# Three expert tiles without tokens move from the end of the plan to places 1, 3 and 5, and two PSUM banks change roles

## The chip, the cores and the metric

The kernel runs on one core of one Trainium2 chip. The metric is the device time of one execution in microseconds (us). Below, the engines are called PE (TensorE, matrix products), ACT (ScalarE), DVE (VectorE), POOL (GpSimd) and SP (SyncE, which only issues transfers here).

## The reference

Three stages run one after the other: windowed causal attention, a dense block with h - tanh(h), and a mixture of eight experts in which every token goes to one expert. Cut to what matters:

```python
# q, k, v: (4, 8, 576, 64); keys from 63 back to the query itself
attn = softmax(q @ k.T / 8, masked to 0 <= i - j < 64) @ v
x = attn as (2304, 512)
h = x @ w_in                        # 512 -> 2048
x = (h - tanh(h)) @ w_out           # 2048 -> 512
# mixture: 8 experts, one for each token
logits = cosine(x, expert_emb) / tau
expert_idx = argmax(logits); gate = softmax(logits)[expert_idx]
for e in range(8):
    mask = expert_idx == e
    hid = maximum(x[mask] @ w1[e], 0)          # 512 -> 1024
    out[mask] = gate[mask] * (hid @ w2[e])     # 1024 -> 512
```

## The kernel before

Every product is made of three fp32r products (high by high, high by low, low by high; `products`, L1159 to L1164), so each operand is first split into a high part (ACT, a cast) and a low part (DVE, a subtraction).

The first two stages take some 570 us and are one interleaved schedule; they are touched only in POOL's `constants(2)` (L508 to L518), which makes small tables while `w_in` is being split.

The third stage is the one that the change is about. Tokens are routed to slots of a table in DRAM, sorted by expert. Each expert's tokens are cut into tiles of 128, the last one padded. The number of tiles in the program is fixed at NTILE = (2304 + 8 * 127) // 128 = 25, enough for the worst routing. How many of them hold tokens depends on the inputs. A plan made by DVE (L986 to L1015) says for each place s of the 25: which expert (`plan[0]`), whether the expert changes at s (`plan[1]`), which of two weight slots is used (`plan[2]`), and whether the tile is live, that is, has tokens (`plan[3]`). Before, all live tiles come first. `rows` (L1000), used by an indirect load on POOL (L566), says where in the table the tokens of each place stand. A place without tokens reads rows that hold the index T, a padding row.

The loop over places (`experts`, L295) is unrolled for s = 0 to 3 and from 20 on, and a hardware loop of four places a round between. In step s each engine does, in this order:

- PE: the first product of s (24 matmuls, or for a tile that is not live only waits and two semaphore increments, L1323 to L1328); transposes of the gathered tokens of s+1 (L1294); the second product of s-1 (24 matmuls, or a wait and an increment); eight transposes of `hid` of s (L1340).
- ACT: `hTh` of s-1, rounding of `w2` of s and of `w1` of s+1 when the expert changes there (L689, four pieces), `relu` of s (L734), `xgh` of s+1 (L754), the scaled result `y` of s-1 (L764).
- DVE: `hTl` of s-1 (L1055), the low parts of `w2` of s and `w1` of s+1 (L966), `take_ids` of s+2 (L1031, L1032), `xgl` of s+1 (L1063).
- POOL: the scatter of `y` of s-2 to the output (L587), the gather of the tokens of s+2 (L577), which waits for `take_ids` of s+2.
- SP: `fetch(s)`: 4 transfers of `w1` and 4 of `w2`, carried out only where the expert changes at s. Each waits until the same piece of place s-1 has been split (or been passed over).

Each engine works its list strictly in order. Only the two matrix products are left out for a tile that is not live: gather, transposes, `relu`, splits, `y` and scatter are done for all 25.

The experts of the 22 live tiles here change at live tiles 2, 4, 7, 11, 15, 17 and 19 (counted from 0): these are the places at which ACT rounds new weights. The places 22, 23 and 24 have no tokens.

Of the kernel before, what the change touches and what calls it, by code (L numbers as in the profile page):

```python
# [9 lines left out]
ALU = mybir.AluOpType  # L10
AX = mybir.AxisListType.X
ds = bass.ds

P = 128
# [20 lines left out]
def build(nc, q, k, v, w_in, w_out, emb, tau, w1, w2, out):  # L35
    B, H, S, D = q.shape
    T, DM, F = B * S, H * D, w_in.shape[1]
    E, _, F2 = w1.shape
    KC, FC, F2C = DM // P, F // P, F2 // P

# [15 lines left out]
    NTILE = (T + E * (P - 1)) // P  # L56
    REGION = T
    ROWS = E * REGION + P
# [6 lines left out]
    with ExitStack() as ctx:  # L65
        def sb(name, shape, dt=F32, scope=ctx):
            return scope.enter_context(nc.sbuf_tensor(name, shape, dt))

        def sem(name):
            return ctx.enter_context(nc.semaphore(name))  # L70

        def sems(name, n):
            return [sem(f"{name}{i}") for i in range(n)]

        banks = ctx.enter_context(nc.psum_tensor("banks", [P, 8, BANK], F32))
# [21 lines left out]
        plan = sb("plan", [P, 4, NTILE], I32)  # L97
        tiles18 = sb("tiles18", [P, E, MAXT])
        tri8 = sb("tri8", [P, E, E])
        jcol = sb("jcol", [P, NTILE])  # L100
        pcol = sb("pcol", [P, 1])
        notfirst = sb("notfirst", [P, E])
        changes = sb("changes", [P, NTILE + 1])
        en1 = sb("en1", [E, 3])
        enroot = sb("enroot", [E, 1])

# [60 lines left out]
        phase2 = ctx.enter_context(ExitStack())  # L167
# [23 lines left out]
        ended = sb("ended", [P, NTILE, E], scope=phase2)  # L191
        moved = sb("moved", [P, NTILE, E], scope=phase2)
        c8 = [sb(f"c8_{i}", [P, E], scope=phase2) for i in range(8)]
        experts_ended = sb("experts_ended", [P, NTILE], scope=phase2)
        row = [sb(f"row{i}", [P, 1], scope=phase2) for i in range(2)]
        rows = sb("rows", [P, 1], I32, phase2)

        mstep, dstep = sem("mstep"), sem("dstep")
        ident_made, masks_made, pads_zeroed, consts_made = sem("ident_made"), sem("masks_made"), sem("pads_zeroed"), sem("consts_made")
# [23 lines left out]
        rows_planned, tabs_loaded, tabs_transposed, ids_ready, ids_taken = (sem(n) for n in (  # L223
            "rows_planned", "tabs_loaded", "tabs_transposed", "ids_ready", "ids_taken"))
# [35 lines left out]
        psJ = banks[:, 0, :]  # L260
        psG = [banks[:, i, :] for i in (0, 1)]
        psHT = [banks[:, i, :] for i in (2, 3)]
        psY = [banks[:, i, :] for i in (4, 6)]
        psXG = banks[:, 5, :]

        q_blocks = q.rearrange("b h (i p) d -> p (b h i) d", p=WINDOW)
        k_blocks = k.rearrange("b h (i p) d -> p (b h i) d", p=WINDOW)
# [45 lines left out]
        def chained(eng, semaphore, base=0):  # L313

            done = [0]

            def then(instruction):
                done[0] += 1
                instruction.then_inc(semaphore, 1)
                eng.wait_ge(semaphore, base + done[0])  # L320
            return then
# [124 lines left out]
        def _(pool):  # L446

            alone = chained(pool, mstep)
            alone(pool.memset(ident[:], 0.0))
            alone(pool.affine_select(out=ident[:], in_=ident[:], compare_op=ALU.not_equal, fill=1.0, base=0,  # L450
                                     pattern=[[-1, P]], channel_multiplier=1))
# [3 lines left out]
            for h in range(2):  # L455
                m = mask[h * WINDOW:(h + 1) * WINDOW]
                alone(pool.affine_select(out=m, in_=m, compare_op=ALU.is_ge, fill=MASKED, base=-1,
                                         pattern=[[1, P]], channel_multiplier=-1))
                alone(pool.affine_select(out=m, in_=m, compare_op=ALU.is_ge, fill=MASKED, base=WINDOW,
                                         pattern=[[-1, P]], channel_multiplier=1))  # L460
# [32 lines left out]
            def constants(part):  # L493
                if part == 0:
                    alone(pool.memset(power[:], 0.5))
                    alone(pool.memset(plain_ones[:], 1.0))
                    alone(pool.affine_select(out=plain_tri[:], in_=plain_ones[:], compare_op=ALU.is_gt, fill=0.0, base=0,
                                             pattern=[[1, P]], channel_multiplier=-1))
                    alone(pool.memset(added[:], 0.0))
                    for exact, plain in ((ones, plain_ones), (tri, plain_tri), (running, added)):  # L500
                        alone(pool.tensor_copy(exact[:], plain[:]))
                if part == 1:
                    for st in range(ST):

                        alone(pool.iota(pair[st][:, 0:1], [[0, 1]], base=P * st - TB, channel_multiplier=1, allow_small_or_imprecise_dtypes=True))
                    alone(pool.iota(em8[:], [[0, ST], [1, E]], base=-E, channel_multiplier=0, allow_small_or_imprecise_dtypes=True))
                    alone(pool.iota(rowbase[:], [[0, ST], [REGION, E]], base=0, channel_multiplier=0, allow_small_or_imprecise_dtypes=True))
                if part == 2:  # L508
                    alone(pool.iota(tiles18[:], [[0, E], [P, MAXT]], base=0, channel_multiplier=0, allow_small_or_imprecise_dtypes=True))
                    alone(pool.memset(tri8[:], 1.0))  # L510
                    alone(pool.affine_select(out=tri8[:], in_=tri8[:], compare_op=ALU.is_ge, fill=0.0, base=0,
                                             pattern=[[1, E], [-1, E]], channel_multiplier=0))
                    alone(pool.iota(jcol[:], [[1, NTILE]], base=0, channel_multiplier=0, allow_small_or_imprecise_dtypes=True))
                    alone(pool.iota(pcol[:], [[0, 1]], base=0, channel_multiplier=1, allow_small_or_imprecise_dtypes=True))
                    alone(pool.memset(notfirst[:], 1.0))
                    alone(pool.memset(notfirst[:, 0:1], 0.0))
                    alone(pool.memset(changes[:, 0:1], 0.0))
                    pool.sem_inc(consts_made, 1)  # L518

            def scatter_slots(m):  # L520
                pool.wait_ge(slotted, m + 1)
                pool.wait_ge(table_cleared, 32)
                for st in range(ST):
                    pool.indirect_dma_start(out=table, out_offset=bass.IndirectOffsetOnAxis(ap=slot[:, st:st + 1], axis=0),
                                            in_=pair[st][:], in_offset=None).then_inc(scattered, 16)

            constants(0)
            for j in range(FIRST + 5):
                if 3 <= j < FIRST + 3:
# [12 lines left out]
            for n in range(NBLK):  # L542
                for c, s in steps(n):
                    if n == 0 and c + 2 < FC:
                        split_w_in(c + 2)
                    pieces(s)
                    pieces(s + 1)
                    if n == 0 and c in (3, 5):
                        constants(1 if c == 3 else 2)
                    if n == 0 and c == 6:  # L550
                        pool.wait_ge(en_squared, 1)
                        pool.tensor_tensor(enroot[:], en1[:, 0:1], power[0:E, 0:1], ALU.pow).then_inc(en_rooted, 1)
                    if n > 0 and c == 9:
                        pool.wait_ge(squared, ST * n)
                        pool.tensor_tensor(norm[:], ss[:], power[:], ALU.pow).then_inc(rooted, 1)
                    if n > 0 and c == 12:
                        scatter_slots(n - 1)
# [223 lines left out]
        def _(dve):  # L781
# [203 lines left out]

            dve.wait_ge(totals_ready, 1)  # L986
            then = chained(dve, planstep)
            count, tiles, ends, moves, starts, filled, passed, jumped = (t[:] for t in c8)
            then(dve.tensor_copy(count, psN))
            then(dve.tensor_tensor(cmp18[:], count.unsqueeze(2).broadcast_to((P, E, MAXT)), tiles18[:], ALU.is_gt))  # L990
# [1 line left out]
            then(dve.tensor_tensor(prod8[:], tiles.unsqueeze(1).broadcast_to((P, E, E)), tri8[:], ALU.mult))  # L992
            then(dve.tensor_reduce(ends, prod8[:], AX, ALU.add))
            then(dve.tensor_scalar(moves, tiles, -float(P), float(REGION), ALU.mult, ALU.add))
            then(dve.tensor_scalar(passed, ends, pcol[:, 0:1], None, ALU.is_le))
            then(dve.tensor_tensor(jumped, passed, moves, ALU.mult))
            then(dve.tensor_reduce(row[0][:], jumped, AX, ALU.add))
            then(dve.tensor_scalar(row[1][:], row[0][:], 1.0 / P, pcol[:, 0:1], ALU.mult, ALU.add))

            dve.tensor_scalar(rows[:], row[1][:], float(E * REGION // P), None, ALU.min).then_inc(rows_planned, 1)  # L1000


            then(dve.tensor_tensor(ended[:], jcol[:].unsqueeze(2).broadcast_to((P, NTILE, E)), ends.unsqueeze(1).broadcast_to((P, NTILE, E)), ALU.is_ge))
            then(dve.tensor_reduce(experts_ended[:], ended[:], AX, ALU.add))
            then(dve.tensor_scalar(plan[:, 0, :], experts_ended[:], float(E - 1), None, ALU.min))
            then(dve.tensor_tensor(starts, ends, tiles, ALU.subtract))
            then(dve.scalar_tensor_tensor(out=filled, in0=tiles, scalar=0.0, in1=notfirst[:], op0=ALU.is_gt, op1=ALU.mult))
            then(dve.tensor_tensor(ended[:], jcol[:].unsqueeze(2).broadcast_to((P, NTILE, E)), starts.unsqueeze(1).broadcast_to((P, NTILE, E)), ALU.is_ge))
            then(dve.tensor_tensor(moved[:], ended[:], filled.unsqueeze(1).broadcast_to((P, NTILE, E)), ALU.mult))
            then(dve.tensor_reduce(changes[:, 1:NTILE + 1], moved[:], AX, ALU.add))  # L1010
            then(dve.tensor_tensor(plan[:, 1, :], changes[:, 1:NTILE + 1], changes[:, 0:NTILE], ALU.subtract))
            then(dve.tensor_copy(plan[:, 2, :], changes[:, 1:NTILE + 1]))
            then(dve.tensor_scalar(plan[:, 2, :], plan[:, 2, :], 1, None, ALU.bitwise_and))
            then(dve.tensor_scalar(plan[:, 3, :], jcol[:], ends[:, E - 1:E], None, ALU.is_lt))
            dve.sem_inc(planned, 1)  # L1015
            low_first_w1([0])

# [383 lines left out]
```

## Time and profile before

| | us |
|---|---|
| median of 3 runs | 893.06 |
| lowest, highest | 890.51, 893.79 |
| the profiled execution, its own time | 894.78 |
| span in its trace | 893.0 |
| PE busy in the span | 831.4 (93%) |
| ACT busy, DVE busy | 362.3 (41%), 398.3 (45%) |
| mean granted clock, as a share of 2.4 GHz | 0.964 |

All times inside the trace are counted from the start of the span. The time lies 1.8 us above the span. A row of the timeline gives the start, the duration, the engine and line, the operation, the tile that it writes and those that it reads, the number of instructions merged, and in brackets the idle time before it with what ended it. SPq and POOLq are issues of transfers.

### The profile page before, as it was taken

The page shows a single profiled execution, that of the slowest core. Times are in us where ns is not written, and L with a number is a line of the kernel's source. Part 1 is how long each engine was busy: PE and PEld are TensorE (multiplying, and loading weights), DVE is VectorE, ACT ScalarE, POOL GpSimd, SP SyncE. Part 2 cuts the span into 40 slices and gives each one's busy share as a digit, 9 for nine tenths or more (in the row PEclk, how much of TensorE's full clock was granted, in tenths as well). Part 3 has the DMA queues.
Part 4 walks back from the last instruction along what each step waited for, and adds up shares of the span by engine and source line. Part 5 has one row for each costly group of instructions (what it writes and reads, how often), then busy time and mean ns, then how long its engine had stood idle before and what let it go on. Part 6 is the DMA issues. An engine that isn't in the chain of part 4 may idle for free. (4 is left out here: it accounts for less than half of the span.)

```text
span 893.0 us, 16016 instructions
## 1 busy us (share of the span) xinstructions
PE 831.4 (93%) x4496; PEld 727.1 (81%) x4497; DVE 398.3 (45%) x1205; ACT 362.3 (41%) x880; POOL 201.7 (23%) x288
## 2 busy tenths in 40 slices
PE   3679999999999999999999999668999999999992
PEld 3679998889999989988889999557888888888871
DVE  3436655445444544444443333555435251455412
ACT  2525554333433343334333222515535262555423
POOL 2636651112111211121112001120111111111111
PEclk9879999999999999999999999869999999999996
DMA  5494112211211112112003400116634251655210
GB/s 126 106 277 128 39 45 63 69 26 32 56 55 24 34 41 78 40 27 79 23 1 56 168 2 0 36 37 213 228 124 142 85 182 41 235 212 214 60 38 23
DMA packets 101299, 77.34 MB, mean 87 GB/s; under 512 B 79132, under 2 KB 80289, under 8 KB 101234
## 3 DMA queue, kind: packets, MB, share of 16 engines
q1 hardware_dynamic: 96610, 65.20, 24.7%
q0 software_dynamic: 4624, 11.32, 4.1%
q8 instruction: 34, 0.56, 0.3%
q14 instruction: 31, 0.25, 0.1%
HBM read 142.39 MB, written 11.44 MB: 172 GB/s over the span
## 5 line engine op out<-in xcount | busy, mean ns | idle before, releaser
L1162 PE MATMUL banks<-xh,win_h 128*128 128x384 f32 x384 | 137.4, 358 | 1.8 <-POOL xl L482 1.8
L1164 PE MATMUL banks<-xh,win_l 128*128 128x384 f32 x384 | 130.8, 341 | 0.0
L1163 PE MATMUL banks<-xl,win_h 128*128 128x384 f32 x384 | 130.4, 340 | 0.0
L870 DVE TENSOR_TENSOR gf<-banks,gf 128x384 f32<-128x384 f32 x96 | 53.5, 557 | 157.3 <-ACT gf L652 157.3
L652 ACT ACTIVATE gf<-banks 128x384 f32<-128x384 f32 x96 | 47.2, 491 | 184.2 <-PE banks L1164 184.2
L1162 PE MATMUL banks<-wout_h,gh 128*128 128x512 f32 x288 | 119.1, 414 | 0.0
L1164 PE MATMUL banks<-wout_h,gl 128*128 128x512 f32 x288 | 113.7, 395 | 0.0
L1163 PE MATMUL banks<-wout_l,gh 128*128 128x512 f32 x288 | 112.7, 391 | 0.0
L472 POOL TENSOR_TENSOR sm<-sm,rr 128x384 f32<-128x384 f32 x48 | 41.9, 874 | 305.7 <-DVE rr L821 305.7
L874 DVE TENSOR_TENSOR gl<-gf,gh 128x384 fp32r<-128x384 f32 x96 | 55.1, 574 | 112.7 <-ACT gh L659 108.1
L659 ACT CAST gh<-gf 128x384 fp32r<-128x384 f32 x96 | 49.2, 512 | 128.9 <-PE banks L1164 127.7
L1162 PEld LDWEIGHTS banks<-xh,win_h 128*128 128x128 f32 x384 | 73.3, 191 | 2.7 <-POOL xl L482 2.1
L1163 PEld LDWEIGHTS banks<-xl,win_h 128*128 128x128 f32 x384 | 73.4, 191 | 0.6
L1055 DVE TENSOR_TENSOR hTl<-banks,hTh 128x512 fp32r<-128x512 f32 x50 | 32.3, 686 | 92.2 <-ACT hTh L745 92.1
L1164 PEld LDWEIGHTS banks<-xh,win_l 128*128 128x128 f32 x384 | 73.2, 191 | 0.0
L1162 PE MATMUL banks<-w1h,xgh 128*128 x176 | 71.2, 404 | 2.1 <-DVE xgl L1063 1.0
L1162 PE MATMUL banks<-w2h,hTh 128*128 x176 | 70.8, 402 | 0.9 <-DVE hTl L1055 0.9
L1164 PE MATMUL banks<-w1h,xgl 128*128 x176 | 69.2, 393 | 0.0
L1164 PE MATMUL banks<-w2h,hTl 128*128 x176 | 68.9, 391 | 0.0
L1163 PE MATMUL banks<-w1l,xgh 128*128 x176 | 68.7, 390 | 0.0
L1163 PE MATMUL banks<-w2l,hTh 128*128 x176 | 68.6, 390 | 0.0
L607 ACT ACTIVATE sm<-sm,nmx 128x128 f32<-128x128 f32 x144 | 55.8, 391 | 21.0 <-DVE nmx L810 20.9
(185 smaller groups left out, 1487.4 us busy)
## 6 DMA issues: line engine op xcount, KB each, us to landing
w1raw<-in_moe_w_dram SPq DMA_DIRECT2D x104, 512.0 KB
w2raw<-in_moe_w_dram SPq DMA_DIRECT2D x104, 512.0 KB
vw<-in_v_dram SPq DMA_DIRECT2D x48, 96.0 KB, 2.7
x_rows<-x SPq DMA_DIRECT2D x6, 768.0 KB, 3.8
wout_raw<-in_moe_w_out_dram SPq DMA_DIRECT2D x4, 1024.0 KB, 6.8
win_raw<-in_moe_w_in_dram SPq DMA_DIRECT2D x3, 1024.0 KB, 8.2
qk<-in_q_dram SPq DMA_DIRECT2D x30, 96.0 KB, 2.7
qk<-in_k_dram SPq DMA_DIRECT2D x30, 96.0 KB, 2.7
```

The source lines that it names most:

```text
L472: pool.tensor_tensor(sm[g % 4][:], sm[g % 4][:], rr[:, g % 4, :].unsqueeze(2).broadcast_to((P, GB, P)), ALU.mult).then_inc(normed, 1)
L607: last = act.activation(sm[g % 4][:, u, :], sm[g % 4][:, u, :], ACT.Exp, bias=nmx[:, g % 4, u:u + 1], scale=-1.0, accum_out=rs[:, g % 4, u ...
L652: act.activation(gf[c % 2][:], psH[c % 2], ACT.Tanh).then_inc(tanh_ready, 1)
L659: act.copy(gh[c % 2][:], gf[c % 2][:]).then_inc(g_high, 1)
L870: dve.tensor_tensor(gf[c % 2][:], psH[c % 2], gf[c % 2][:], ALU.subtract).then_inc(g_ready, 1)
L874: dve.tensor_tensor(gl[c % 2][:], gf[c % 2][:], gh[c % 2][:], ALU.subtract).then_inc(g_split, 1)
L1055: dve.tensor_tensor(hTl[:, part, :], psHT[half].rearrange("p (k t) -> p k t", k=KC), hTh[:, part, :], ALU.subtract).then_inc(hT_split, 1)
L1162: pe.matmul(to, sh, mh, start=start, stop=False)
L1163: pe.matmul(to, sh, ml, start=False, stop=False)
L1164: return pe.matmul(to, sl, mh, start=False, stop=stop)
```

## The change

The plan counts the tiles without tokens (`idle_tiles` = 25 less the live ones). Place j is idle if j is odd and fewer than `idle_tiles` odd places lie before it; `place_of[j]` is j less the idle places up to j, and takes the place of j in all comparisons with the experts' ends and starts. With 3 idle tiles these are the places 1, 3 and 5. They keep the expert of the live tile before them. A row of an idle place is pushed beyond the table's last region by adding ROWS before the minimum, so that it still reads padding. The order of the live tiles stays. The live tiles 0, 1, 2, 3, 4, 5, ... stand at the places 0, 2, 4, 6, 7, 8, ..., so that the expert changes at the places 4, 7, 10, 14, 18, 20 and 22.

POOL makes two more tables. The chain of DVE between the token counts and `rows` gets six more instructions, and the rest of the plan up to `planned` three more. The PSUM bank of the odd tiles' second product becomes 5 in place of 6, and the one of the transposed tokens 6 in place of 5. Nothing in the loop over the places is edited.

```diff
-        psY = [banks[:, i, :] for i in (4, 6)]
-        psXG = banks[:, 5, :]
+        psY = [banks[:, i, :] for i in (4, 5)]
+        psXG = banks[:, 6, :]
...
+                    alone(pool.iota(halves[:], [[1, (NTILE + 1) // 2], [0, 2]], base=0, channel_multiplier=0, allow_small_or_imprecise_dtypes=True))
+                    alone(pool.memset(odd_rows[:], 1.0))
+                    for i in range(2):
+                        alone(pool.affine_select(out=odd_rows[:, i, :], in_=odd_rows[:, i, :], compare_op=ALU.is_ge, fill=0.0, base=i - 2,
+                                                 pattern=[[-2, (NTILE + 1) // 2]], channel_multiplier=1))
...
+            then(dve.tensor_reduce(idle_before_row[:], odd_rows[:], AX, ALU.add))
...
-            then(dve.tensor_scalar(passed, ends, pcol[:, 0:1], None, ALU.is_le))
+            then(dve.tensor_scalar(idle_tiles[:], ends[:, E - 1:E], -1.0, float(NTILE), ALU.mult, ALU.add))
+            then(dve.tensor_scalar(row_idle[:], idle_before_row[:], idle_tiles[:, 0:1], None, ALU.min))
+            then(dve.tensor_tensor(place_of_row[:], pcol[:], row_idle[:, 1:2], ALU.subtract))
+            then(dve.tensor_tensor(row_is_idle[:], row_idle[:, 1:2], row_idle[:, 0:1], ALU.subtract))
+            then(dve.tensor_scalar(passed, ends, place_of_row[:, 0:1], None, ALU.is_le))
...
-            then(dve.tensor_scalar(row[1][:], row[0][:], 1.0 / P, pcol[:, 0:1], ALU.mult, ALU.add))
-            dve.tensor_scalar(rows[:], row[1][:], float(E * REGION // P), None, ALU.min).then_inc(rows_planned, 1)
-            then(dve.tensor_tensor(ended[:], jcol[:].unsqueeze(2).broadcast_to((P, NTILE, E)), ends.unsqueeze(1).broadcast_to((P, NTILE, E)), ALU.is_ge))
+            then(dve.tensor_scalar(row[1][:], row[0][:], 1.0 / P, place_of_row[:, 0:1], ALU.mult, ALU.add))
+            then(dve.scalar_tensor_tensor(out=row[2][:], in0=row_is_idle[:], scalar=float(ROWS), in1=row[1][:], op0=ALU.mult, op1=ALU.add))
+            dve.tensor_scalar(rows[:], row[2][:], float(E * REGION // P), None, ALU.min).then_inc(rows_planned, 1)
+            then(dve.tensor_scalar(idle[:], halves[:], idle_tiles[:, 0:1], None, ALU.min))
+            then(dve.tensor_tensor(place_of[:], jcol[:], idle[:, 1:NTILE + 1], ALU.subtract))
+            then(dve.tensor_tensor(is_idle[:], idle[:, 1:NTILE + 1], idle[:, 0:NTILE], ALU.subtract))
+            then(dve.tensor_tensor(ended[:], place_of[:].unsqueeze(2).broadcast_to((P, NTILE, E)), ends.unsqueeze(1).broadcast_to((P, NTILE, E)), ALU.is_ge))
...
-            then(dve.tensor_scalar(plan[:, 3, :], jcol[:], ends[:, E - 1:E], None, ALU.is_lt))
+            then(dve.tensor_scalar(plan[:, 3, :], is_idle[:], -1.0, 1.0, ALU.mult, ALU.add))
```

## Rows read from the trace of the kernel before

**Rows 1.** The page's costliest groups: one of the expert products

```profile
L1162 PE MATMUL banks<-w1h,xgh 128*128 x176 | 71.2, 404 | 2.1 <-DVE xgl L1063 1.0
```

**Rows 2.** PE's timeline from the third stage's start: start us, duration

```profile
592.54 2.06 PE L1277 MATMUL banks<-w1h,ones 128*128 128x512 f32 x4
...
601.17 1.07 PE L1340 MATMUL banks<-ident,hid 128*128 128x128 f32 x8
...
615.86 1.14 PE L1340 MATMUL banks<-ident,hid 128*128 128x128 f32 x8 [0.91 <-ACT hid L734]
...
618.01 0.49 PE L1162 MATMUL banks<-w1h,xgh 128*128 x1 [1.01 <-issue]
...
629.52 1.03 PE L1340 MATMUL banks<-ident,hid 128*128 128x128 f32 x8
...
641.81 1.03 PE L1340 MATMUL banks<-ident,hid 128*128 128x128 f32 x8
642.60 0.47 PE L1162 MATMUL banks<-w1h,xgh 128*128 x1
```

**Rows 3.** The timeline of all engines around the last live tile

```profile
868.83 0.97 POOL L577 DMA_INDIRECT xg<-x_rows,ids  x1 [3.01 <-DVE ids L1032]
...
871.21 0.69 ACT L764 ACTIVATE y<-banks,gate 128x512 f32<-128x512 f32 x1 [2.20 <-PE banks L1164]
...
872.98 0.66 PE L1294 MATMUL banks<-ident,xg 128*128 128x128 f32 x4 [0.93 <-DMA xg<-x_rows,ids]
873.05 1.02 POOL L587 DMA_INDIRECT out_dram<-y,ids  x1 [3.25 <-issue]
```

**Rows 4.** The chain that ended last: start us, us, what

```profile
882.43 0.70 DVE hTl L1055
...
884.73 0.98 POOL out_dram L587
```

**Rows 5.** The answer on the output tensor: how long its scatters take

```profile
DMA to landing us min/median/max: 2.1/2.8/5.5
```

**Rows 6.** The other engines' timeline in the third stage's first steps

```profile
599.81 0.95 POOL L577 DMA_INDIRECT xg<-x_rows,ids  x1 [8.24 <-DVE ids L1032]
...
617.23 1.09 ACT L745 CAST hTh<-banks 128x512 fp32r<-128x512 f32 x2
...
618.35 3.90 ACT L689 CAST w2h<-w2raw 128x1024 f32 x4
...
619.85 4.63 DVE L966 TENSOR_TENSOR w2l<-w2raw,w2h 128x1024 f32 x4 [0.69 <-ACT w2h L689]
...
624.40 0.15 DVE L1031 COPY gate<-gates_all 128x1 f32<-128x1 f32 x1
...
626.54 2.47 SPq L414 DMA_DIRECT2D w1raw<-in_moe_w_dram  x4
...
633.21 3.90 ACT L689 CAST w1h<-w1raw 128x1024 f32 x4 [1.85 <-issue]
```

**Rows 7.** DVE's and POOL's timeline while the plan is made

```profile
578.05 0.15 DVE L1000 TENSOR_SCALAR rows<-row 128x1 int32<-128x1 f32 x1
...
581.36 0.24 DVE L1014 TENSOR_SCALAR plan<-jcol,c 128x25 int32<-128x25 f32 x1
...
583.62 0.97 POOL L566 DMA_INDIRECT tabs<-slots,rows  x1 [4.71 <-issue]
```

**Rows 8.** POOL and PE in the dense stage's first block

```profile
87.18 1.30 POOL L491 TENSOR_TENSOR win_l<-win_raw,win_h 128x512 fp32r<-128x512 f32 x1
...
94.50 0.42 PE L1162 MATMUL banks<-xh,win_h 128*128 128x384 f32 x1
```

**Rows 9.** Windows: stretch, busy times by engine, granted clock, DMA share, GB/s

```profile
596.00:596.25 0.25, 0.25 (x3) 0.21 (x2) 0.25 (x1) 0.00 (x0) 0.00 (x0) 0.92 0.00 0
...
617.00:618.00 1.00, 0.00 (x1) 0.00 (x0) 0.63 (x2) 1.00 (x3) 0.92 (x1) 1.00 0.17 64
...
875.75:876.00 0.25, 0.25 (x4) 0.18 (x3) 0.00 (x0) 0.25 (x2) 0.00 (x0) 0.86 0.00 0
```

More of the change, by code:

```diff
@@ L103, in build @@
         changes = sb("changes", [P, NTILE + 1])
+        halves = sb("halves", [P, NTILE + 1])
+        odd_rows = sb("odd_rows", [P, 2, (NTILE + 1) // 2])
         en1 = sb("en1", [E, 3])
@@ L194, in build @@
         experts_ended = sb("experts_ended", [P, NTILE], scope=phase2)
-        row = [sb(f"row{i}", [P, 1], scope=phase2) for i in range(2)]
+        row = [sb(f"row{i}", [P, 1], scope=phase2) for i in range(3)]
         rows = sb("rows", [P, 1], I32, phase2)
+        idle_before_row = sb("idle_before_row", [P, 2], scope=phase2)
+        idle = sb("idle", [P, NTILE + 1], scope=phase2)
+        is_idle = sb("is_idle", [P, NTILE], scope=phase2)
+        row_is_idle = sb("row_is_idle", [P, 1], scope=phase2)
+        idle_tiles = sb("idle_tiles", [P, 1], scope=phase2)
+        place_of_row = sb("place_of_row", [P, 1], scope=phase2)
+        place_of = sb("place_of", [P, NTILE], scope=phase2)
+        row_idle = sb("row_idle", [P, 2], scope=phase2)
         mstep, dstep = sem("mstep"), sem("dstep")
@@ L1007, in _ @@
             then(dve.scalar_tensor_tensor(out=filled, in0=tiles, scalar=0.0, in1=notfirst[:], op0=ALU.is_gt, op1=ALU.mult))
-            then(dve.tensor_tensor(ended[:], jcol[:].unsqueeze(2).broadcast_to((P, NTILE, E)), starts.unsqueeze(1).broadcast_to((P, NTILE, E)), ALU.is_ge))
+            then(dve.tensor_tensor(ended[:], place_of[:].unsqueeze(2).broadcast_to((P, NTILE, E)), starts.unsqueeze(1).broadcast_to((P, NTILE, E)), ALU.is_ge))
             then(dve.tensor_tensor(moved[:], ended[:], filled.unsqueeze(1).broadcast_to((P, NTILE, E)), ALU.mult))
```

## The prediction

> **What bounds the kernel now.** I read the page first: PE is busy 93% of the span, and each of the eight matmul groups of the expert stage has 176 members [rows 1]. A live tile has 8 of each group (4 pieces of the contraction by 2 halves), so 22 tiles are live and 25 - 22 = 3 places are idle: the change does act on these inputs. Then PE's timeline: once the stage runs, the transposes of `hid` of one live tile begin 12.29 us after those of the one before (629.52, 641.81), with no idle time between. So PE sets the pace there, and it is 0.79 us from these eight transposes to the next product (641.81 to 642.60); the four of `xg` are half of that, 0.4, and each of the two products is (12.29 - 0.8 - 0.4) / 2 = 5.6 us [rows 2]. Last, the timeline around the end and the chain that ended last. The last live tile's `y` is scaled at 871.21 and its scatter goes out at 873.05; then three idle places still follow one another through transposes, `relu`, split, `y` and scatter, and the last scatter goes out at 884.73 [rows 3, 4]. That is 11.7 us in which no expert product runs. At the front PE loses a little too: before the third live tile it waits 0.91 and 1.01 us for work behind the first newly loaded weights [rows 2].
>
> **What it takes away.** The tail of idle places: 884.73 - 873.05 = 11.7 us [rows 3, 4]. The live tail stays as it was, since the last live tile's second product had an idle place behind it before as well. An idle scatter writes nothing and a live one does, and landings range from 2.1 to 5.5 with a median of 2.8 [rows 5]; I take 0.2 us of loss there, from 0 to 0.7 (2.8 - 2.1).
>
> **What it adds in front.** An idle place leaves out two products, which are what hides the other engines' work, and leaves in everything else. I follow the clock of the trace of before, with these pieces: a gather takes 872.98 - 868.83 = 4.1 us from issue until PE transposes [rows 3]; a half of `relu` or `hTh` 0.6, `xgh` 0.6 (1.09 for two halves [rows 6], the others taken alike), `y` 0.7 [rows 3], a split on DVE 0.7 [rows 4]; four pieces of weights are rounded in 3.9 us, and their low parts are done 619.85 + 4.63 - 618.35 = 6.15 us after the rounding began, with `take_ids` right behind (624.40) [rows 6].
>
> Step 1 is idle. The gather of place 2 goes out at 599.81, so PE, done with `hid` of tile 0 at 602.24 [rows 2, 6], waits until 603.9, and the second product of place 0 starts at 604.5 (0.4 of transposes, 0.2 to start). Step 2 is live, expert unchanged: 5.6 + 0.8, first product from 610.9 to 616.5. Step 3 is idle: ACT must do half of `relu` (617.2), `xgh` (617.8), `y` (618.5) and half of `hTh` (619.1), DVE a half of `hTl` (619.8), and the second product of place 2 starts at 620.2 and ends at 625.8.
>
> Meanwhile the first new weights, now for place 4, are late. SP may fetch `w1` of place 4 only when DVE has passed over place 3, in its step 2, at about 614, and issues near 616.2. From the issue at 626.54 to the rounding's start at 633.21 was 6.7 us, and its last piece did not wait [rows 6], so by 623 to 624 the pieces are there. ACT comes to them at 619.6 + 1.85 (the pause before the same rounding, 633.21 [rows 6]) = 621.5, ends at 625.4 and only then does `relu` (626.5); DVE ends at 621.5 + 6.15 = 627.6, then `take_ids` and `xgl`, 628.5. So first product of place 4 at about 629.0, to 634.6. It stands behind three queues here (ACT's rounding, DVE's low parts, then `xgl`), as it did before, but with 5.6 us less of products over it.
>
> Step 4 rounds `w2` of place 4: ACT after `xgh`, `y` and `hTh` of place 3 at 629.5; DVE's low parts end at 635.6. Behind them in DVE's queue is `take_ids` of place 6, behind that POOL's gather (636.0), which lands at 640.1. Place 5 is idle and covers nothing: the second product of place 4 starts at 640.7 instead of near 636, and ends at 646.3. Place 6, live, has its first product from 647.1 to 652.7, and place 7 changes expert once more: ACT begins at 648.2 + 2.1 = 650.3, DVE ends at 656.5, `xgl` 657.4, first product of place 7 at 657.9.
>
> Place 7 is live tile 4. Before, its first product started at 642.60 [rows 2]. The state behind it is the same, so the front costs 657.9 - 642.6 = 15.3 us. Of this, 3 x (0.8 + 0.4) = 3.6 are transposes of idle places, the rest are waits. The lower bound takes 3.4 us for a gather (its 0.97 of issue, then 2.4; the first gathers of the stage are no more exact) and with it 13.5; the upper one takes 1 us more for each of two places at which gather and weights share the DMA engines, 17.3. After place 7 no idle place follows, and the pace is 12.3 again.
>
> **What it adds elsewhere.** The six instructions before `rows` and three more before `planned` are short like those around them: (581.36 - 578.05) / 12 = 0.28 us each, and 0.15 to 0.24 where they are as small as L1000 and L1014, so 1.3 and 1.9 us. `rows` comes at 578.2, but the load that uses it goes out at 583.62, held by the slot scatters [rows 7], so 4 us hide it. `planned` moves from 581.6 to 583.5; of those who wait for it, SP's first fetches are held by DVE's low parts anyway, and PE is in its warming matmuls. I take 0; with the cover gone it is 1.9. POOL's four extra instructions take about 1 us: they stand before the split that ends at 88.5, and PE starts on those columns at 94.50 [rows 8], so 6 us hide them, and 1 us is the price otherwise. The banks change roles only between stages whose reads are long over: 0.
>
> **The clock.** After the last dense product ended at 871.0, the granted clock stayed full through sparse transposes until 875.75 to 876.00, where it fell (0.86 is the mix) to 1.2 GHz, 4.9 us later; it did not fall in the 3.1 us between the products around 615.86 and 618.01 (1.00). It came back at about 596.0, after matmuls running from 592.54 and some before [rows 2, 9]; half speed over 3.5 to 4.2 us costs 1.7 to 2.1 us. After the change the distances between dense products are 3.8 (step 1), 3.7 (step 3), 3.2, 6.1 (step 5) and 5.2 (step 7). The 6.1 is longer than the one that lost the clock, the 5.2 is on the edge, the others are nearer the one that kept it. So I count one loss, 2.0 us, with bounds of none and two (4.1).
>
> The Trainium skill ("TensorE: Matmul & The Clock Gate", "HAM oscillation — how this bites in real kernels") says that waits between bursts of matmuls send the array back to half clock, and that this is paid again at each wait. The trace agrees that a sparse stretch does it (875.75 [rows 9]); that waits as short as 3.7 us do, no row here shows. By that page the waits in steps 1 and 3 would be paid as well.
>
> **The sum.** -11.7 + 0.2 + 15.3 + 2.0 = +5.8 us. The profiled execution took 894.78, 1.7 above the median of 893.06; on the median the sum gives 898.9.
>
> **The rivals.**
> Clock kept: the same without the 2.0, +3.8, 896.9. For it speaks that transposes run inside each gap; against it, they ran in the tail too.
> Clock lost at the four long gaps: +3.8 + 4 x 2.0 = +11.8, 904.9. Against it: the gap at 615.86 kept its clock with almost as much sparse time. This is what the cited page would make of it.
> Faster, because the idle steps are hidden: they give SP time, and the weights that PE waited for before (0.91 + 1.01) come under other work. If PE lost only the 3.6 us of transposes and won the 1.9, the sum were -11.7 + 0.2 + 3.6 - 1.9 = -9.8, 883.3. It needs the gathers to be back before PE asks, and ACT's rounding not to stand before `relu`; the order of the lists speaks against it. It decides the sign from a front cost below 11.5 us, and makes 0.5% from one below 7.
> The plan is exposed: `planned` or `rows` late by 1.9 with everything else as above, +7.7, 900.8. The 4 us before the load at 583.62 speak against it.
> That nothing changes (no idle tile) is excluded by [rows 1].
>
> **How the numbers follow.** One loss of clock 0.33 (898.9), clock kept 0.22 (896.9), two to four losses 0.17 (900.9 to 904.9), plan exposed 0.05, a front cost of 7 to 11.5, as between the hidden case and mine, 0.11 (888.6 to 893.1), hidden 0.12 (about 883 to 888). What a measurement of this kernel can tell from no change is 0.5%, 4.5 us: below 888.6 or above 897.5. Faster is the hidden case, 0.12. Slower takes the losses of clock and the exposed plan, 0.55, less a tenth of them for a front at its lower bound, plus a tenth from the clock-kept case at its upper: 0.52. The rest, 0.36, is the same. The range leaves out most of the hidden case below and the four losses above: 889 to 904. The likeliest's own range is 897 to 901 by the bounds of the front.
>
> **What would show it.** In the trace after: the last scatter within 2 us of the last live `y`, and no sparse stretch of three steps before it; the first product of the fifth live tile near 658; PE idle before `xg` at steps 1 and 5, ended by the gather; ACT's first `w1` rounding at about 621 to 622 without a wait for DMA, and PE's transposes of `hid` waiting for `relu` behind it; `tabs` still loaded at about 583.6; the clock below 1.00 in the stretch 640 to 645. The prediction is wrong if gathers come back well before 4 us, if the unchanged steps' pauses on ACT and DVE are longer than I took (then each idle step costs more), or if the clock is lost at every gap.

## The result and the profile after

The changed kernel takes 908.03 us (median of 4, 905.57 to 911.48) against 893.15 for the kernel before: ratio 1.0173, 95% interval 1.015 to 1.0195. The forecast was 898.9, with a range of 889 to 904. The direction was right, the size was not: 14.9 us instead of 5.8.

PE's timeline of the changed kernel over the first steps of the expert stage, cut to the rows that matter, which answers to [rows 2]. The transposes of `xg` (gathered tokens) are L1319 here, those of `hid` L1365; a row of L1187 is the first of the 24 matmuls of a product.

```profile
600.71 0.60 PE L1319 MATMUL banks<-ident,xg 128*128 128x128 f32 x4
601.15 1.07 PE L1365 MATMUL banks<-ident,hid 128*128 128x128 f32 x8
604.00 0.66 PE L1319 MATMUL banks<-ident,xg 128*128 128x128 f32 x4 [1.77 <-DMA xg<-x_rows,ids]
605.61 0.69 PE L1187 MATMUL banks<-w2h,hTh 128*128 x1 [0.96 <-issue]
612.80 1.03 PE L1365 MATMUL banks<-ident,hid 128*128 128x128 f32 x8
619.13 0.60 PE L1319 MATMUL banks<-ident,xg 128*128 128x128 f32 x4
619.57 1.07 PE L1365 MATMUL banks<-ident,hid 128*128 128x128 f32 x8
622.91 1.11 PE L1319 MATMUL banks<-ident,xg 128*128 128x128 f32 x4 [2.27 <-DMA xg<-x_rows,ids]
624.55 0.79 PE L1187 MATMUL banks<-w2h,hTh 128*128 x1 [0.52 <-issue]
632.48 1.03 PE L1365 MATMUL banks<-ident,hid 128*128 128x128 f32 x8
638.84 0.60 PE L1319 MATMUL banks<-ident,xg 128*128 128x128 f32 x4
639.57 1.09 PE L1365 MATMUL banks<-ident,hid 128*128 128x128 f32 x8
645.97 1.11 PE L1319 MATMUL banks<-ident,xg 128*128 128x128 f32 x4 [5.32 <-DMA xg<-x_rows,ids]
647.84 0.79 PE L1187 MATMUL banks<-w2h,hTh 128*128 x1 [0.76 <-issue]
656.08 1.03 PE L1365 MATMUL banks<-ident,hid 128*128 128x128 f32 x8
662.44 0.60 PE L1319 MATMUL banks<-ident,xg 128*128 128x128 f32 x4
664.60 1.09 PE L1365 MATMUL banks<-ident,hid 128*128 128x128 f32 x8 [1.56 <-ACT hid L750]
667.25 0.79 PE L1187 MATMUL banks<-w1h,xgh 128*128 x1 [1.56 <-DVE xgl L1088]
```

The idle steps 1, 3 and 5 begin behind the transposes of `hid` at 601.15, 619.57 and 639.57. With its first product left out, PE waits there for gathered tokens: 1.77, 2.27 and 5.32 us. Then comes one second product, and these last too long: 605.61 to 612.80 is 7.2 us, 624.55 to 632.48 is 7.9, 647.84 to 656.08 is 8.2, where 5.6 is the length at full clock. The windows say why. Their columns are the stretch, its length, the busy times of PE, its weight loads, DVE, ACT and POOL, the granted clock, the DMA share and GB/s. The first four stretches are those three products and the beginning of place 7's first one, the last is a piece of the first:

```profile
605.60:612.80 7.20, 7.19 (x25) 5.75 (x25) 0.91 (x3) 0.91 (x2) 0.94 (x1) 0.76 0.14 36
624.50:632.50 8.00, 7.95 (x25) 6.34 (x26) 5.62 (x7) 4.61 (x6) 0.96 (x1) 0.68 0.97 365
647.80:656.10 8.30, 8.27 (x25) 6.51 (x26) 0.62 (x1) 0.00 (x0) 0.44 (x1) 0.65 0.77 284
667.20:673.00 5.80, 5.75 (x18) 4.65 (x19) 5.32 (x6) 4.36 (x5) 1.91 (x2) 0.71 0.19 62
608.50:609.00 0.50, 0.50 (x2) 0.39 (x2) 0.00 (x0) 0.00 (x0) 0.00 (x0) 0.50 0.74 197
```

The granted clock, third number from the right, is 0.76, 0.68, 0.65 and 0.71 on average: each of the four runs for some time at 1.2 GHz (0.50 in the last row) and gets 2.4 back on the way.

What DVE and POOL do ahead of the longest wait:

```profile
636.26 4.63 DVE L982 TENSOR_TENSOR w2l<-w2raw,w2h 128x1024 f32 x4 [1.09 <-ACT w2h L705]
641.35 0.15 DVE L1056 COPY gate<-gates_all 128x1 f32 x1 [0.46 <-DVEq L1070]
...
642.49 0.97 POOL L593 DMA_INDIRECT xg<-x_rows,ids  x1 [7.22 <-DVE ids L1057]
```

The row numbers for place 6 are taken (`take_ids`) from 641.35 on, behind the low parts of `w2`; the gather leaves at 642.49 and PE can use it at 645.97, 3.5 us later.

The plan's chain, against [rows 7]:

```profile
579.33 0.15 DVE L1022 TENSOR_SCALAR rows<-row 128x1 int32<-128x1 f32 x1
...
583.37 0.18 DVE L1039 TENSOR_SCALAR plan<-is_idle 128x25 int32<-128x25 f32 x1
...
584.18 1.60 POOL L582 DMA_INDIRECT tabs<-slots,rows  x1 [5.22 <-issue]
```

`rows` and the plan come 1.3 and 2.0 us later, and the load that uses `rows` starts 0.6 later. The end, against [rows 3, 4]:

```profile
896.90 0.69 ACT L780 ACTIVATE y<-banks,gate 128x512 f32<-128x512 f32 x1 [6.26 <-PE banks L1189]
898.38 0.98 POOL L603 DMA_INDIRECT out_dram<-y,ids  x1 [6.92 <-ACT y L780]
```

The last live `y` comes 896.90 - 871.21 = 25.7 us later than before, and nothing follows its scatter. The last scatter of all moved from 884.73 to 898.38, 13.65 us, and the span's rest behind it grew from 8.3 to 8.8 us: together the 14.2 us between the spans (907.2, 893.0).

### The profile page after: what moved, and what is told of

The parts are those of the page before. It is cut to its first block and busy times, and to the rows that moved or that the text cites. A ratio compares the mean times of both kernels' runs of the same rounds, so it can differ in the third digit from the quotient of the medians.

```text
span 907.2 us, 16024 instructions
## 1 busy us (share of the span) xinstructions
PE 835.9 (92%) x4496; PEld 729.1 (80%) x4497; DVE 400.0 (44%) x1214; ACT 362.5 (40%) x880; POOL 203.5 (22%) x292
## 5 line engine op out<-in xcount | busy, mean ns | idle before, releaser
L1187 PE MATMUL banks<-xh,win_h 128*128 128x384 f32 x384 | 137.3, 357 | 1.8 <-POOL xl L492 1.8
L1187 PE MATMUL banks<-wout_h,gh 128*128 128x512 f32 x288 | 119.1, 414 | 0.0
L1187 PE MATMUL banks<-w2h,hTh 128*128 x176 | 73.7, 418 | 3.5 <-issue 2.2
L1187 PEld LDWEIGHTS banks<-xh,win_h 128*128 128x128 f32 x384 | 73.3, 191 | 2.7 <-POOL xl L492 2.1
L1187 PE MATMUL banks<-w1h,xgh 128*128 x176 | 71.5, 406 | 2.1 <-DVE xgl L1088 2.1
L1188 PE MATMUL banks<-w2l,hTh 128*128 x176 | 71.2, 405 | 0.0
L1189 PE MATMUL banks<-w2h,hTl 128*128 x176 | 71.2, 404 | 0.0
```

The costliest lines, as they stand in the source:

```text
L1187: pe.matmul(to, sh, mh, start=start, stop=False)
L1188: pe.matmul(to, sh, ml, start=False, stop=False)
L1189: return pe.matmul(to, sl, mh, start=False, stop=stop)
```

## The experiments

Each ratio is against the kernel before, run beside it on the same chip; 0.001 is 0.9 us. In brackets stands its 95% interval. The edits are shown shortened, some in words.

**1. The parts that move no place.** All additions stay, but the idle places are pushed to the end:

```diff
-pool.iota(halves[:], ..., base=0, ...)
+pool.iota(halves[:], ..., base=-20, ...); then max(halves, 0)
-base=i - 2          # odd_rows
+base=i - 42
-plan[3] = 1 - is_idle
+plan[3] = jcol < ends[E - 1]
```

> The changed kernel with all its added instructions, tables and bank roles, but with the three idle places left at the end of the plan (22, 23, 24). Theory of the front (idle places cost PE's waits and its clock in steps 1 to 7): this runs as the kernel before, 893, within 1 us. Rival of the plan and the banks (the added instructions, the later load of the token table or the banks cost several us): 896 to 900. The trace after shows the load of the token table only 0.6 us later, so I expect 893 to 894.

0.9994 (0.9981 to 1.0007). Tables, nine instructions and the banks' roles together cost nothing that can be measured. The whole difference comes from where the idle places stand.

**2. What the idle tail is worth.** The kernel before with `NTILE = 22`.

> The kernel before with 22 places in all instead of 25, so that there is no idle place at all (it leaves out nothing for these inputs, but would not hold every routing). It measures what the idle tail is worth: my sum says 11.7 us less a slower last landing of 0.2 to 0.7: 881.5 to 882. A rival, by which the tail of idle places lies partly under the landing of the last live scatter, gives 884 to 886.

0.9855 (0.9817 to 0.9892), 12.9 us (9.6 to 16.3). The term of 11.7 was sound; these few runs can't tell the two apart.

**3. The clock.** Dummy matmuls behind the left-out first product:

```diff
                     pe.sem_inc(hid_ready, 1)
+                    for _ in range(10):
+                        pe.matmul(banks[:, 7, :], ones[:], ones[:].unsqueeze(1).broadcast_to((P, 4, P)), start=True, stop=True)
```

> The changed kernel with ten dummy matmuls of 512 columns (about 2.2 us at full clock) in PE's list at each idle place, before it waits for the next gathered tokens. Theory of the clock (the four products after the gaps ran 1.6, 2.3, 2.6 and 1.6 us too long because the clock had fallen, 8 us in all): if most of the losses are avoided, 908 falls by 4 to 7 us to 901 to 904, with the products back at 5.6 us. Rival (the products are slow for another reason, as memory or bank traffic): they stay slow and the time is 908 or, by the dummies that outlast a wait, 909.

1.012 (1.006 to 1.0181): the sign is as the clock's theory says, but the interval is wide and touches that of the changed kernel (1.015 to 1.0195). The traces are clearer. The windows of this kernel, over the same four products as above:

```profile
602.80:608.30 5.50, 5.50 (x26) 4.51 (x25) 0.69 (x1) 0.58 (x1) 0.94 (x1) 1.00 0.18 48
620.00:625.60 5.60, 5.60 (x28) 4.59 (x27) 5.05 (x7) 4.58 (x6) 0.00 (x0) 1.00 1.02 364
641.10:646.70 5.60, 5.58 (x25) 4.58 (x26) 0.06 (x1) 0.00 (x0) 0.65 (x1) 1.00 0.79 267
657.80:663.50 5.70, 5.66 (x19) 4.58 (x20) 5.21 (x6) 4.35 (x5) 1.90 (x2) 0.74 0.17 51
```

Three products are back at 5.6 us and a clock of 1.00, with the same bank, the same weights and the DMA engines as busy (a share of 1.02 in the second against 0.97): what had slowed them was the clock, and not memory or bank traffic. The fourth, which has no dummies ahead, still pays. From tile 0's first product to the fifth live tile's it is 657.84 - 591.60 = 66.2 us here and 667.25 - 595.12 = 72.1 in the changed kernel, 5.9 less.

With 14 dummies there and 6 behind the left-out second product:

> The changed kernel with fourteen dummy matmuls behind each left-out first product and six behind each left-out second one; nothing else moved. With ten behind the first alone the ratio was 1.012 and one product pair (place 7) still ran at half clock. Theory of the clock: all products of the steps 0 to 7 at full clock, 1.6 us less and the rest as there: 1.010. If the dummies themselves get in the way of the transposes: 1.013 or more.

1.010 (1.0074 to 1.0126), clear of the changed kernel by some 6.5 us. The number is the one that the theory gave, but its reason did not come true: place 7's first product was to run at full clock, and it did not.

```profile
661.80:667.50 5.70, 5.70 (x18) 4.56 (x19) 5.20 (x6) 4.32 (x5) 1.86 (x2) 0.70 0.21 54
```

So the hit is partly luck. Between the two marks it is 661.80 - 593.57 = 68.2 us, 2.0 more than with ten dummies: they take room themselves.

**4. The gathers, two tries that failed.** `take_ids` of s+2 at the head of DVE's step:

```diff
             def expert_step(r, i):
+                take_ids(r, i, 2)
                 low_hT(r, i)
...
-                take_ids(r, i, 2)
```

> The changed kernel with DVE's choice of the row numbers of place s+2 moved to the head of its list in a step, ahead of the low parts of the weights. Theory of the queue (the gather for place 6 is late because its row numbers stand behind 4.6 us of low parts): the wait of 5.3 us before the tokens of place 6 goes, the one of 2.3 us before place 4 shrinks, and the time falls by 5 to 8 us (one lost clock with it), to 900 to 903. Rival (PE would wait there anyway for the hidden tile's split or the weights): less than 2 us.

1.0396 (1.0367 to 1.0426). The same behind `low_hT`:

> The changed kernel with DVE's choice of row numbers for place s+2 between the low part of hid and the low parts of the weights (the first try put it ahead of both, where it waits for a scatter that has not landed and holds everything behind it). Theory of the queue: PE's wait for the tokens of place 6 (5.3 us) falls under 1 us, the product behind it keeps its clock, and the time falls by 6 to 9 us against the changed kernel, to a ratio of 1.007 to 1.011. Rival (the choice is held by the scatter here too): the ratio stays above 1.015 and DVE waits for a landing in each step.

1.0401 (1.038 to 1.0423); and with dummies on top:

> The same order of DVE's list and, at each idle place, ten dummy matmuls behind the left-out first product and six behind the left-out second one. Theory of the clock and the queue together: no product of the first eight steps runs at 1.2 GHz; what stays are the idle places' transposes (3.6 us) and the waits for relu, rounding and splits. I expect a ratio of 1.000 to 1.005 with the kernel before. Rival (most of the front's price is neither clock nor gather): 1.008 or more.

1.0396 (1.0375 to 1.0416). All three are 20 us worse than the changed kernel. The waits of the second try (who for whom: us in total, times, longest):

```profile
DVE gate L1056 <- DMA out_dram<-y,ids: 51.5, 21, 5.9
...
PE banks L1187 <- DVE xgl L1088: 19.1, 7, 6.0
```

`take_ids` reuses a buffer that a scatter still reads. At its old place that scatter has mostly landed (the changed kernel's DVE waits for it at 646.14, for 2.74 us); moved up, DVE waits for it in 21 steps, and everything behind it in the list, low parts and `xgl`, is late for PE. The rival stated for the second try was right; the expectation for the first had not thought of it. These runs say nothing on the gather for place 6.

**5. The gathers, without touching DVE.** Eight places unrolled, and the first ten gathers read the whole table of row numbers:

```diff
-            for i in range(4):
-                step(0, i)
+            for i in range(8):
+                step(i // 4, i % 4)
...
-                hold(pool, ids_taken, s + 1)
+                pool.wait_ge(ids_ready, 1)              # where s < 10
...
-in_offset=bass.IndirectOffsetOnAxis(ap=ids[buf][:, 0:1], axis=0)
+in_offset=bass.IndirectOffsetOnAxis(ap=ids_all[:, s:s + 1], axis=0)
```

> The changed kernel with eight places unrolled before the loop instead of four, and the gathers of the first ten places reading their row numbers straight from the table, so that they don't stand behind DVE's list at all. The tries before moved DVE's choice and made it wait for scatters in every step; this moves no one else. Theory of the gather: PE's waits for tokens (1.8, 2.3 and 5.3 us before places 2, 4 and 6) go; PE then waits for the split of hid instead, 2.0, 2.1 and 4.7 us earlier than now: 8.8 us less, ratio 1.0173 - 0.0099 = 1.007, and lower if fewer clocks are lost. Rival (the gathers are not what PE waits for last): 1.015 or more.

1.0063 (1.0041 to 1.0085), where the control, the same edit on the kernel before, is near 1:

> The kernel before with the unrolled eight places and the direct gathers of the first ten, nothing moved: the control for the run direct_ids. If these edits only take away waits for gathers, and none binds in the kernel before: ratio 0.999 to 1.001. If the unrolling changes the pace by itself, it is off by more than 0.002 and the gathers' share has to be corrected by that.

0.9991 (0.9979 to 1.0004). So earlier tokens take 1.0173 - 1.0063 = 0.011, some 10 us, from the change's cost. PE's timeline at steps 1, 5 and 7 of the run with places moved, then the windows of the products behind:

```profile
598.58 1.07 PE L1370 MATMUL banks<-ident,hid 128*128 128x128 f32 x8
601.15 0.63 PE L1324 MATMUL banks<-ident,xg 128*128 128x128 f32 x4 [1.50 <-DVE xgl L1093]
602.80 0.50 PE L1192 MATMUL banks<-w2h,hTh 128*128 x1 [1.02 <-DVEq L1075]
...
637.43 0.49 PE L1192 MATMUL banks<-w2h,hTh 128*128 x1 [1.02 <-DVEq L1075]
...
650.97 0.60 PE L1324 MATMUL banks<-ident,xg 128*128 128x128 f32 x4
...
655.35 0.79 PE L1192 MATMUL banks<-w1h,xgh 128*128 x1 [1.45 <-DVE xgl L1093]
```

```profile
602.80:608.40 5.60, 5.60 (x24) 4.61 (x25) 0.91 (x3) 1.14 (x3) 0.00 (x0) 1.00 0.00 1
637.40:644.60 7.20, 7.17 (x24) 5.74 (x25) 0.81 (x3) 1.35 (x3) 0.30 (x1) 0.76 0.51 167
655.30:661.00 5.70, 5.65 (x18) 4.56 (x19) 5.36 (x6) 4.64 (x5) 1.78 (x2) 0.71 0.39 135
```

No wait for tokens is left, but each idle step still has one of 1.4 to 1.6 us for `xgl` or PE's own sequencer, and 1.02 before the product. All four gaps between dense products are shorter (4.7, 4.5, 4.7 and 4.4 us), and two of the four clock losses are gone. But they are not gone by length alone: the shortest, 650.97 to 655.35, still lost it. With dummies on top:

> The same with ten dummy matmuls behind each left-out first product and six behind each left-out second one. Theory of clock and gather together: 1.007 less some 0.006 to 0.008 for the clock: 0.999 to 1.002. Rival (clock and gather don't add up, since the dummies fill waits that are gone): 1.005 or more, with PE's transposes of hid starting later than in the run without dummies.

1.0059 (1.0035 to 1.0084): this missed. In its trace the four products run at full clock, but the stretch between the two marks is 653.70 - 590.06 = 63.6 us, against 655.35 - 592.59 = 62.8 without dummies: what the clock gives back the dummies take, as the rival said. (Counted on to the next transposes of `hid`, behind the last slow product, the two runs are 75.1 and 75.8 us.)

**6. The price of a place.** Lists of places written into the two tables in place of 1, 3, 5 (in words):

```diff
-halves[k] = k // 2
+halves[k] = number of idle places below k, from the list     # memsets
```

First places 9, 14 and 23, each between live neighbours:

> The changed kernel with the idle places at 9, 14 and 23 in place of 1, 3 and 5: apart from each other and not next to a change of expert. Theory: an idle place there costs 1.2 us of transposes and 1.0 to 1.5 us of waiting for the split of hid, its neighbours are live and cover gather and relu, and the clock stays full; 3 x 2.5 = 7.5 us against the 11.7 of the tail: ratio 0.995 (about 887). Rival (an idle place costs 5 us or more wherever it stands, since the products that it leaves out hide the other engines' work): 1.004 or more.

1.0014 (1.0002 to 1.0026): neither theory's number. PE's timeline around place 9:

```profile
700.02 1.03 PE L1370 MATMUL banks<-ident,hid 128*128 128x128 f32 x8
...
722.87 0.60 PE L1324 MATMUL banks<-ident,xg 128*128 128x128 f32 x4
```

Without an idle place the `xg` transposes of the step after next begin, at the pace of [rows 2], 12.29 + 6.36 = 18.65 us after the `hid` transposes (6.36 is a block of `hid` transposes and a first product, 0.79 and 5.57). It takes 22.85, so an idle place costs 4.2 us here, with the clock at 1.00 throughout; I had said 2.5. At the end it costs 3.9. Moving it gains nothing even where it harms least.

One idle place at 14, two at the end, so that live tile 15's new weights come two places behind it:

> Only one idle place moved, to 14, the other two at the end. Theory: minus one third of the tail (3.9 us) plus 2.5 us: ratio 0.998. Rival of the same price everywhere (5 us or more): 1.001 or more. The trace is to show how long PE goes without a dense product around place 14: 3 us or less and a granted clock of 1.00.

1.0051 (1.0033 to 1.007), where my theory said 0.998: the rival holds. It is worse than three spaced ones.

```profile
760.24 1.03 PE L1370 MATMUL banks<-ident,hid 128*128 128x128 f32 x8
...
778.20 1.96 PE L1370 MATMUL banks<-ident,hid 128*128 128x128 f32 x8 [3.02 <-ACT hid L755]
788.00 0.60 PE L1324 MATMUL banks<-ident,xg 128*128 128x128 f32 x4
```

The same distance is 27.76 us, a price of 9.1: `relu` stands behind the rounding of the new `w1` (3.02), which the left-out products no longer cover, and the clock goes (the transposes take 1.96). Nor was the stretch without a dense product 3 us or less, as expected, but 6.5 (774.58 to 781.05). Place 1 alone:

> Only one idle place moved, to 1; the other two at the end. Theory (the front's price adds up place by place): the changed kernel lost 2 to 3 us of waiting, 1.2 of transposes and 1.6 of clock at place 1, less the 1.0 that the kernel before waits there too, against 3.9 of tail: +0 to +2 us, ratio 1.000 to 1.002. Rival (the first new weights come one place later in this order, so that the idle place hides the wait for them): 0.997 or less. Other rival (any idle place ahead of the new weights makes their whole chain late): 1.005 or more.

1.0031 (1.0018 to 1.0044), between the theory (up to 1.002) and the last rival (1.005 or more), so some 6.7 us for the place, in place of the 3.9 in the tail. Its trace shows the clock lost after place 1 and again behind the new weights, where PE waits for `relu` and `xgl`:

```profile
615.99 0.60 PE L1324 MATMUL banks<-ident,xg 128*128 128x128 f32 x4
617.78 1.14 PE L1370 MATMUL banks<-ident,hid 128*128 128x128 f32 x8 [1.19 <-ACT hid L755]
620.33 0.79 PE L1192 MATMUL banks<-w1h,xgh 128*128 x1 [1.41 <-DVE xgl L1093]
```

Three such places at the front cost 25.7 us, 8.6 each.

**7. The tail itself.** The kernel before, with `relu`, the split of `hid` and its transposes passed over at an idle place (`If` on `plan[3]`, increments in the `Else`):

> The kernel before (idle places at the end), in which ACT, DVE and PE pass over relu, the split of hid and its transposes at an idle place, with semaphore increments in their stead; gather, split of the tokens, scaling and scatter stay. The tail is 11.7 us now and the run without any idle place was 12.9 us faster. Theory (the tail is the chain relu, transposes, split of each idle place): it shrinks to about 6 us, ratio 0.994. Rival (the added branches cost the live places as much, or the chain of branches alone takes 3.9 us a place): 1.000 or more.

1.0008 (0.9993 to 1.0023). The scatter of the last live tile and that of the last idle one:

```profile
870.48 1.02 POOL L587 DMA_INDIRECT out_dram<-y,ids  x1 [2.52 <-issue]
...
882.00 0.98 POOL L587 DMA_INDIRECT out_dram<-y,ids  x1 [1.96 <-ACT y L776]
```

11.5 us, as before (11.7). Leaving out that work alone, at the price of a test and a branch on each engine, shortens the tail by nothing that counts. Whether the branches cost as much as the work or the work was never in the way, this run can't tell. Then every engine leaves the whole step:

```diff
             for s in range(4 * rounds, NTILE + 1):
-                step(s // 4, s % 4)
+                with eng.If(eng.value_load(plan[0:1, 3, ds(s - 1, 1)], min_val=0, max_val=1)):
+                    step(s // 4, s % 4)
```

and likewise SP's `fetch(s)` under the test of s, POOL's scatter under that of s-2 and its gather under that of s-1, with the final waits inside.

> The kernel before, in which every engine passes over a whole step from step 20 on when the tile of the step before it is idle, so that the three idle places at the end cost one test of a register each; SP waits for its transfers before the next fetch there. It still holds every routing. Theory (the tail is the chain from engine to engine, mostly branches and register loads, not the work in it): the time comes close to the run without any idle place (ratio 0.9855), 0.985 to 0.989. Rival (the tests themselves, about 1 us each on every engine, make a chain as well): 0.995 or more.

0.989 (0.987 to 0.991), 881.94 us. By the ratios it beats the kernel before by 10 us and the changed one by 25. The last scatter of its trace, in the chain that ended last:

```profile
869.94 1.01 POOL out_dram L600
```

It is the last live tile's, with no idle one behind it. The span ends at 880.7, 10.8 us later, where it was 8.3 in the kernel before and in the run with 22 places: that is most of the 3 us by which this run stays above the latter. Only this routing was run; that the edit holds the others follows from its tests and wasn't measured.

## Why the prediction was wrong, by its own steps

**What bounds, and the tail taken away** (-11.7 + 0.2): right. Without idle places the kernel gains 12.9; the changed kernel has none of that tail.

**The front at full clock** (15.3): right in kind and nearly in size. The last live `y` is 25.7 us late; the four slow stretches are 1.6 + 2.4 + 2.7 + 1.6 us too long (the last from 667.25 to the next transposes of `hid`), two blocks of `xg` transposes 0.5 each, 9.3 in all; that leaves 16.4. Most waits stand where the prediction put them: tokens of places 2 and 6, `relu` behind the rounding and `xgl` behind the low parts at place 7. The wait for the tokens of place 4 is one that it did not have. The gather for place 6 was to leave at 636.0 and left at 642.5, since the steps ahead had run late, and took 3.5 us instead of 4.1. The slow products hide part of this: the wait of 2.4 us before the first product of place 4 (629.0 in the forecast, less 625.8 and 0.8) didn't appear; the product ahead of it ended only at 632.48 and lasted 2.4 longer. ACT's first rounding for place 4 began at 623.29 in place of 621.5 and waited three times for its transfers, 1.2 us in all; this too the slow product hid. The lower bound of 13.5 doesn't come out of its own pieces: 0.7 less for each of the two gathers on the path gives 13.9.

**The clock** (2.0): this step failed. I put the gaps between dense products at 3.8, 3.7, 3.2, 6.1 and 5.2 us and counted one loss of the clock, 2.0 us. The gaps were 4.9, 5.4, none, 9.0 and 4.8, all four lost the clock, and together this cost 9.3 us. Two errors led there. First, the two short gaps came out too short, by 1.1 and 1.7 us. I gave PE 0.2 us to start the product behind the tokens where it idles 0.5 to 1.0 (605.61, 624.55, 647.84). And the gather for place 4 is missing from the working: DVE comes to its row numbers only at 618.06, 2.6 us after the low part of `hid`, and PE waits for the tokens until 622.91. Second, I drew the line at the one gap that I had seen lose its clock, with nothing measured between 3.1 and 4.9. The rival "clock lost at the four long gaps" (904.9; two to four losses had 0.17 of the chance) is what happened. It is 3.1 us short of the median: 1.3 for its 2.0 a loss, which was 2.3 on average, 1.1 for the front, and the rest is the difference between the profiled execution and the median. In the same way the forecast of +5.8 becomes the +14.2 between the two spans: 7.3 by the clock, 1.1 by the front. Dummies in the gaps took 4.7 us off by the ratios and 5.9 by the traces, of the 7.7 that the three losses in their reach had cost.

The rule of the Trainium skill that stood beside it ("TensorE: Matmul & The Clock Gate", "HAM oscillation — how this bites in real kernels"), that each wait between bursts is paid anew, is borne out by these four products, though not by every run: of the four gaps between dense products in the run `direct_ids`, 4.4 to 4.7 us long, two kept the clock. Weighed higher than one gap of the trace before, the rule would have moved the likeliest case to 905.

**Plan, tables, banks** (0): right, 0.9994. **The clock kept, the hidden case, the exposed plan:** none of them occurred. The faster rival fails on what it named itself: the gathers were not back and the rounding stood before `relu`.

**What stays open.** Why each execution of the changed kernel differs more than one of before (905.57 to 911.48; the slowest had the lowest mean clock, 0.954) wasn't tried beyond that. The start of the stage moves from trace to trace as well: tile 0's first product starts between 590.1 and 595.1, which is why stretches between two marks are compared above. In what parts the 3.9 us of an idle place in the tail divide between branches, register loads, gathers and the work itself is not shown. Shown is only that passing over `relu`, transposes and split by branches gains nothing, and that passing over whole steps does.

## What to carry to other kernels

A placeholder in a pipeline costs what its neighbours no longer hide: here 4.2 us between live tiles, 9.1 ahead of a change of weights, 8.6 each for the three at the front, 3.9 at the end, although its own work on PE is 1.2. Before an empty unit of work is moved, ask what the work that it leaves out was covering, and count the clock for every stretch that it makes sparse, including those just above the longest that is known to be safe. The better edit here is to leave out the empty steps altogether: it was worth 10 us.

## What the runs showed of the hardware

**Gaps between dense products, and the clock.** A gap is counted from the end of one product's matmuls to the start of the next product; 8 to 16 transposes lie in it. Without dummies, these were measured:

| run | kept the clock, us | lost it, us |
|---|---|---|
| before | 3.1 | |
| `spaced` | up to 3.3 (767.88 to 771.19) | |
| `direct_ids` | 4.7 (598.14 to 602.80), 4.5 (614.74 to 619.27) | 4.7 (632.72 to 637.43), 4.4 (650.97 to 655.35) |
| `one_at_1` | | 5.1 (597.37 to 602.51), 4.3 (615.99 to 620.33) |
| after | | 4.9, 5.4, 9.0, 4.8 |
| `one_at_14` | | 6.5 (774.58 to 781.05) |

From 4.3 to 4.7 us the length alone doesn't say what happens. Dummies don't settle it either: `warm_both` lost the clock at its last gap (656.99 to 661.80) and `direct_warm` kept it (648.90 to 653.70), both 4.8 us long with six dummies at the start. Nor need the clock fall inside the gap: in `direct_ids` the product at 637.43 began at 1.00, and the fall came behind its start.

```profile
637.50:638.00 0.50, 0.50 (x3) 0.41 (x4) 0.00 (x0) 0.50 (x2) 0.20 (x1) 1.00 0.06 16
638.00:638.50 0.50, 0.50 (x3) 0.41 (x2) 0.00 (x0) 0.50 (x2) 0.00 (x0) 0.57 0.26 41
```

A loss costs 1.5 to 2.8 us of product time. It isn't the longer gap that costs more: 2.7 us after 9.0, but 2.8 after the 4.3 of `one_at_1` (620.33 to the next transposes of `hid` at 634.61, 14.3 us in place of 11.5).

**An in-order list.** A wait put ahead of other work on DVE in 21 steps, 2.5 us each on average, cost 20 us, more than the whole change: the wait is passed on to all that stands behind it in the list.
